# Handing tap products to the Pool engine in a fused convolution and two-layer feed-forward kernel

## The reference

```python
w = np.exp(weight_gen - max); w = w / (sum(w) + 1e-9)          # over the 7 taps
x_unf = x_pad[:, idx, :]...                                    # 7 tokens, this one and 6 before
x = np.einsum('bshk,bskhg->bshg', w, x_unf).reshape(B * S, D)  # 24 channels of each head
h = x @ w_in;  x = np.maximum(0.01 * h, h) @ w_out
h = x @ w_in2; r = np.maximum(h, 0.0); out = (r * r) @ w_out2
```

## Time and profile before

| | |
|---|---|
| median of three runs | 1122.15 us (1121.98, 1122.15, 1123.47) |
| the profiled execution | 1122.14 us, its span 1120.2 us |
| PE busy | 1114.8 us, 100% of the span |
| DVE, ACT, POOL busy | 873.2, 656.3 and 7.9 us |
| first matmul of the first `up` | at 11.30 us |

### The profile page before, as it was taken

How to read it: one execution, slowest core, us unless ns; L and a number is a source line. 1 busy time by engine, 2 the same in 40 slices (tenths; PEclk the granted TensorE clock), 3 DMA queues, 4 the chain that set the end, 5 groups by cost and what they waited for, 6 DMA issues and landing times.

```text
span 1120.2 us, 22873 instructions
## 1 busy us (share of the span) xinstructions
PE 1114.8 (100%) x9924; PEld 1108.4 (99%) x9924; DVE 873.2 (78%) x1051; ACT 656.3 (59%) x786; POOL 7.9 (1%) x14
## 2 busy tenths in 40 slices
PE   9999999999999999999999999999999999999998
PEld 8999999999999999999999999999999999999998
DVE  8898886978869787796877869778697786975575
ACT  6666656466565655655656565664656656566564
POOL 2000000000000000000000000000000000000000
PEclk9999999999999999999999999999999999999999
DMA  5311010100102001020010200102001020000001
GB/s 163 107 56 54 12 57 2 43 28 14 56 1 58 12 15 55 3 59 10 15 55 6 58 8 16 54 6 59 7 15 54 11 56 5 16 15 15 1 1 29
DMA packets 81059, 36.54 MB, mean 33 GB/s; under 512 B 58436, under 2 KB 78530, under 8 KB 80960
## 3 DMA queue, kind: packets, MB, share of 16 engines
q1 hardware_dynamic: 80960, 35.10, 11.9%
HBM read 23.25 MB, written 6.29 MB: 26 GB/s over the span
## 4 chain that ended last, share of the span: by engine, by line
PE 99%; DVE 0%; DMA 0%; ACT 0%; issue 0%; ACTq 0%; DVEq 0%
PE h_pair L1133 46%; PE y_main_psum L1178 31%; PE y_rest_psum L1182 21%; PE h_pair L1075 0%; PE h_pair L1142 0%; DMA tap_logits<-in_weight_gen_dram 0%; PE y_main_psum L1075 0%; DVE tap_product L725 0%; PE y_rest_psum L1206 0%; PE h_pair L1227 0%; DVE x_windows L949 0%; ACT x_windows L588 0%; ACT x_parts L491 0%; DVE tap_sum L705 0%; ACT tap_exp L485 0%
## 5 line engine op out<-in xcount | busy, mean ns | idle before, releaser
L1133 PE MATMUL h_pair<-x_parts,w_in_parts 64*128 64x512 f32 x4590 | 565.1, 386 | 0.0
L1133 PEld LDWEIGHTS h_pair<-x_parts,w_in_parts 64*128 64x128 f32 x4590 | 518.7, 184 | 1.7 <-issue 0.2
L1178 PE MATMUL y_main_psum<-g_hi,w_out_parts 64*128 64x512 f32 x2040 | 437.5, 386 | 0.0
L905 DVE TENSOR_TENSOR g_lo<-g,g_hi 128x1024 fp32r<-128x1024 f32 x255 | 311.1, 1220 | 126.1 <-ACT g_hi L574 96.0
L562 ACT ACTIVATE g_hi<-h_pair 128x1024 fp32r<-128x1024 f32 x126 | 129.6, 1029 | 191.8 <-PE h_pair L1133 191.7
L574 ACT ACTIVATE g_hi<-g 128x1024 fp32r<-128x1024 f32 x127 | 134.8, 1061 | 170.5 <-DVE g L896 170.5
L1178 PEld LDWEIGHTS y_main_psum<-g_hi,w_out_parts 64*128 64x128 f32 x2040 | 231.3, 184 | 0.8 <-issue 0.2
L1182 PE MATMUL y_rest_psum<-g_hi,w_out_parts 64*128 64x512 f32 x1020 | 218.7, 386 | 0.0
L1178 PE MATMUL y_main_psum<-g_lo,w_out_parts 64*128 64x512 f32 x1020 | 218.7, 386 | 0.0
L1182 PE MATMUL y_rest_psum<-g_lo,w_out_parts 64*128 64x512 f32 x1020 | 218.6, 386 | 0.0
L896 DVE SCALAR_TENSOR_TENSOR g<-h_pair,u 128x1024 f32<-128x1024 f32 x127 | 155.2, 1222 | 37.8 <-ACT u L568 36.0
(11 more groups left out here) (121 smaller groups left out, 428.6 us busy)
## 6 DMA issues: line engine op xcount, KB each, us to landing
x_windows<-in_x_dram SPq DMA_DIRECT2D x12, 960.0 KB
out_dram<-raw_w_in SPq DMA_DIRECT2D x360, 16.0 KB, 1.5
raw_w_in<-tap_product SPq DMA_DIRECT2D x336, 16.0 KB, 1.8
raw_w_out<-in_moe_w_out_dram SPq DMA_DIRECT2D x16, 192.0 KB, 3.9
tap_logits<-in_weight_gen_dram SPq DMA_DIRECT2D x16, 112.0 KB, 3.0
raw_w_in<-in_moe_w_in_dram SPq DMA_DIRECT2D x8, 192.0 KB, 3.4
raw_w_in<-in_moe_w_in_dram SPq DMA_DIRECT2D x8, 128.0 KB, 3.1
x_windows<-in_x_dram SPq DMA_DIRECT2D x2, 384.0 KB, 4.9
```

Source lines behind the costliest of these rows:

```text
L905: dve.tensor_tensor(GL[n % 4][:, :, :], gate[n % 2][:, :, :], GH[n % 4][:, :, :].bitcast(fp32), ALU.subtract).then_inc(glo_ready, 1)
L1133: last = pe.matmul(h[:, i, :], w[r, slot, a, c], v[r, slot, b, :], start=first, stop=end)
L1178: return pe.matmul(ym[rows][:, :], w[r, c], g[r, i, :], start=start, stop=stop)
```

## The change

Six things change. (1) POOL computes the weights of its own three taps of chunk 0, after DVE's reciprocal; DVE computes six of the seven weights for itself, and no longer the three for POOL. (2) For chunk 1 POOL makes the products of taps 6, 5 and 4 and adds them up in `SECOND[1]` (three products, two adds); DVE makes the four others and adds them in `SECOND[0]`, and at the end adds POOL's sum to it. The order of these operations in the steps of segment 0 is new. (3) `turn_second` turns one sum in place of two. (4) The main part of chunk 0's turned input is rounded half by ACT and half by DVE (`first_x_hi`). (5) The idle pair after the third turned product goes; the one at the end of `turn_first` stays. (6) The first two softmax operations of chunk 1 move on DVE from ahead of `in_lo(0)` to behind `in_lo(1)`.

```diff
+    POOL_SECOND = 3
+    SECOND_OPS = [("times", K - 1 - POOL_SECOND, 0)]
+    for t in range(K - 2 - POOL_SECOND, -1, -1):
+        SECOND_OPS += [("times", t, 2), ("plus", 0, 2)]
+    SECOND_OPS += [("plus", 0, 1)]
...
+            pool.wait_ge(ident_step, 4)
+            pool.wait_ge(conv_op, SOFT - 1)
+            which = slice(min(POOL_TAPS), K, 2)
+            pool.tensor_tensor(tap_w[:, :, which], tap_exp[:, :, which],
+                               tap_rec[:, :].unsqueeze(2).broadcast_to((P, TH, len(POOL_TAPS))), ALU.mult).then_inc(pool_weights, 1)
...
+            pool.wait_ge(x_hi_by_dve, 1)
             pool.tensor_copy(X[0][HP:P, 2, 0, :], X[0][0:HP, 0, 0, :]).then_inc(x_hi_spread, 1)
 
             pool.wait_ge(x_hi_spread, 2)
+            pool.wait_ge(first_loaded[1], 16)
+            pool.wait_ge(first_rest_turned, 1)
+            pool.wait_ge(conv_op, before(1) + SOFT)
+            for i in range(POOL_SECOND):
+                t = K - 1 - i
+                if i:
+                    pool.wait_ge(pool_second, 2 * i - 1)
+                pool.tensor_tensor((prod[1][:, :] if i else SECOND[1]).rearrange("p (a g) -> p a g", g=G),
+                                   xwin[1][:, t * D:(t + TPC) * D].rearrange("p (a g) -> p a g", g=G),
+                                   tap_w[:, :, t].unsqueeze(2).broadcast_to((P, TH, G)), ALU.mult).then_inc(pool_second, 1)
+                if i:
+                    pool.wait_ge(pool_second, 2 * i)
+                    pool.tensor_tensor(SECOND[1], SECOND[1], prod[1][:, :], ALU.add).then_inc(pool_second, 1)
...
-                main = X[s % 2][:, 0, 0, :].rearrange("p (a c) -> p a c", a=2)
-                act.activation(main, hb[pair][:, :, 0:QC], ACT.Copy).then_inc(x_hi_done, 1)
+                n = 1 if s == 0 else 2
+                main = X[s % 2][:, 0, 0, 0:n * QC].rearrange("p (a c) -> p a c", c=QC)
+                act.activation(main, hb[pair][:, 0:n, 0:QC], ACT.Copy).then_inc(x_hi_done, 1)
...
-                    weights(tap_w, slice(min(POOL_TAPS), K, 2)).then_inc(pool_weights, 1)
-                    return weights(first_tap_w, slice(0, K))
+                    return weights(first_tap_w, slice(0, K - 1))
...
+                    if b == 1:
+                        dve.wait_ge(pool_second, 2 * POOL_SECOND - 1)
...
+            def first_x_hi():
+                dve.wait_ge(x_turned, 1)
+                dve.tensor_copy(X[0][:, 0, 0, QC:NC], hb[PAIR[("first turn",)]][:, 1, 0:QC]).then_inc(x_hi_by_dve, 1)
...
                 if j == 0:
                     for i in range(2, SOFT):
                         softmax(1, i).then_inc(conv_op, 1)
-                    second_sums(range(2))
+                    second_sums(range(1))
                 if j == 1:
-                    second_sums(range(2, 4))
+                    second_sums(range(1, 2))
                     in_lo(2)
                 if j == 2:
                     out_lo(1)
+                    second_sums(range(2, 4))
+                if j == 3:
                     second_sums(range(4, 6))
-                if j == 3:
-                    second_sums(range(6, 8))
                     in_lo(3)
                 if j == 4:
                     out_lo(2)
-                    second_sums(range(8, len(SECOND_OPS)))
+                    second_sums(range(6, len(SECOND_OPS)))
...
             first_products()
-            for i in range(2):
-                softmax(1, i).then_inc(conv_op, 1)
             in_lo(0)
+            first_x_hi()
             x_lo_main(0, PAIR[("first turn",)])
...
             in_lo(1)
+            for i in range(2):
+                softmax(1, i).then_inc(conv_op, 1)
...
-                    if n in (2, K - 1):
-                        idle(1)
+                idle(1)
...
-                for b in range(2):
-                    last = turn_product(SECOND[b], main, rest, False, b == 0, b == 1)
-                last.then_inc(x_turned, 1)
+                turn_product(SECOND[0], main, rest, False, True, True).then_inc(x_turned, 1)
```

More of the change, by code:

```diff
@@ L251, in conv_two_ffn_kernel @@
         idle_ready = sem("idle_operand_ready")
+        pool_second = sem("pool_second_chunk_op")
+        x_hi_by_dve = sem("first_x_hi_done_by_dve")
         x_turned = sem("x_transposed")
@@ L460, in _ @@
             pool.wait_ge(x_hi_done, 1)
+            pool.wait_ge(x_hi_by_dve, 1)
             pool.tensor_copy(X[0][HP:P, 2, 0, :], X[0][0:HP, 0, 0, :]).then_inc(x_hi_spread, 1)
             pool.wait_ge(x_hi_spread, 2)
+            pool.wait_ge(first_loaded[1], 16)
[11 more added lines that the diff above has]
+                    pool.tensor_tensor(SECOND[1], SECOND[1], prod[1][:, :], ALU.add).then_inc(pool_second, 1)
+            pool.wait_ge(pool_second, 2 * POOL_SECOND - 1)
             pool.wait_ge(conv_op, before(NCH - FIRST_PLACE))
@@ L484, in exp_of @@
                 act.wait_ge(conv_op, before(k) + EXP + 1)
+                if k == 1:
+                    act.wait_ge(pool_weights, 1)
                 act.activation(tap_exp[:, :, 0:K], tap_shift[:, :, :], ACT.Exp).then_inc(exp_done, 1)
@@ L706, in softmax @@
                 if i == 3:
+                    if k == 1:
+                        dve.wait_ge(pool_weights, 1)
                     return dve.reciprocal(tap_rec[:, :], tap_sum[:, :])
@@ L801, in moved_lo @@
                 last.then_inc(moved_taken, 1)
+            def first_x_hi():
+                dve.wait_ge(x_turned, 1)
+                dve.tensor_copy(X[0][:, 0, 0, QC:NC], hb[PAIR[("first turn",)]][:, 1, 0:QC]).then_inc(x_hi_by_dve, 1)
             def x_lo_main(s, pair):
+                if s == 0:
+                    dve.wait_ge(x_hi_by_dve, 1)
                 dve.wait_ge(x_hi_done, 1 if s == 0 else 2 * s + 2)
@@ L1145, in first_up @@
                 pe.wait_ge(x_hi_done, 1)
+                pe.wait_ge(x_hi_by_dve, 1)
                 product(0, 0, 0, start=True)
```

## The result

The changed kernel takes 1128.38 us (median of six runs, 1128.27 to 1129.64) against 1122.30 for the kernel before. The ratio is 1.0055, with a 95% interval of 1.0042 to 1.0068. It is slower by about 6.1 us, clear of the 0.2% that counts here as no change, where I had forecast no change and 0.93 us less. Even the upper end of my range, 1127.3, was too low.

A forecast was written before the change was run, and what follows sets the result against it. PE was taken to bound the kernel. Gains of 0.38 (head), 0.50 (second turn) and 0.05 (third `down`) sum to 0.93 us, from 1122.14 to 1121.2 us; own range 1120.5 to 1122.4, whole range 1120.5 to 1127.3.

The forecast's parts named there:

- What bounds the kernel: PE, busy for the whole span; DVE is not the bound but has no room from 18 to 38 us.
- POOL in segment 0: Chunk 1's three products and two adds on POOL: 8.3 us, ending at 26.4, with over six us of cover.
- first rival: POOL and DVE hold each other up in segment 0, so PE waits: 1125 to 1127 us; chance 0.43.
- three forms: Engines take turns (chance 0.23), DVE always first (0.16), or slowing in part that stays inside the bound (0.04).
- 0.15 us overlap at 5.55: A POOL product started while a DVE operation with two SBUF inputs ran; no wait seen, judged to tell little.
- the clock: Second rival: without the idle pair at 8.57 PE's clock falls during the transposes, +1.95 us, 1123.2 in all; chance 0.04.
- The second turn: Turn of chunk 1: 16 transposes in place of 32, 1.00 becomes 0.50 us on PE's path, gain 0.50.
- The 0.05 at the third `down`: PE's wait for `out_lo(1)` at 26.54 goes, as DVE has two operations fewer ahead of it: 0.05 us gained.
- The head: Start of the kernel up to `first_up`, which starts and ends 0.38 us earlier; between 0.45 earlier and 0.3 later.
- DVE's own head start: Chunk 0's weights on DVE: without POOL's and with 192 elements for 224, the next operation starts 0.23 us earlier.
- POOL's weights: POOL's 128x96 weight operation for chunk 0: 0.35 us estimated, first product starting at 5.75, 0.20 later than before.
- third rival: POOL's third product holds up `in_lo(0)` by 0.3 to 0.4 us, delaying DVE's rounding: 0.38 gone, 1121.6; chance 0.05.

The follow-up runs named there:

- e2: The kernel before plus only POOL's three taps of chunk 1, the new order of DVE's sums and the single turn; 1128.69 us, ratio 1.0055.
- e3: The changed kernel with POOL's five operations on chunk 1 replaced by ten memsets of the same tiles; 1121.55 us, ratio 0.9992.
- e6: The changed kernel with POOL's five operations on chunk 1 replaced by eight copies with one SBUF input each; 1123.76 us, ratio 1.0012.
- e1: The changed kernel without POOL's work on chunk 1, which DVE convolves alone and which is turned as two sums; 1122.32 us, ratio 0.9999.
- e4: The changed kernel with chunk 1 convolved by DVE alone into one sum, one add more, turned once; 1121.47 us, ratio 0.9992.
- e9: The changed kernel with DVE's gate_lo, in_lo and out_lo in segment 0 moved ahead of chunk 1's sums; 1124.53 us, ratio 1.0017.

## Why the prediction was wrong, point by point

**What bounds the kernel** was read rightly, and so was the place of danger: DVE full from 18 to 38 us, with PE waiting for what it makes.

**The step that failed** is "POOL in segment 0": a price of 1.55 us an operation, 8.3 us in all, hidden behind six us of cover, and nothing charged to DVE. In its place the operations took 2.15 to 2.67 us, 12.2 from first start to last end, and DVE lost 1.35 to 1.6 us at each of five meetings, 7 us in all, against 3.8 taken off it. e2 shows that it is this part, e3 and e6 that it is POOL's reading.

I had the mechanism as the first rival, with the right order, and it came out as worked out: `in_lo(2)` at 26.7 (measured 26.48), `out_lo(1)` at 32.1 (31.52), waits of 2.6 and 3.3 (2.2 and 2.8). That it came so near is in part luck: I left out the start-up of 0.13 to 0.15 us that runs beside the other engine, and took 1.55 for an add that ends 1.67 behind DVE. The mistake was the choice. I gave it 0.43 in three forms and the forecast 0.44, on "no run shown decides it". But the kernel itself held a hint that I named and did not weigh: chunk 0's weights for DVE lie in PSUM, and the only stretch in which both engines worked at once was built so. One of those products in the timeline before the change, beside POOL's of 1.55 at 5.55:

```profile
6.62 0.95 DVE L725 TENSOR_TENSOR g<-x_windows,h_pair 128x768 f32<-128x768 f32 x1
```

The absence of slowing there was evidence about DVE operations with one input in SBUF alone. The 0.15 us overlap at 5.55 was too short to speak, since 0.13 to 0.15 us of an operation are start-up that runs beside the other engine anyway.

**The range** failed by a second term that I had at another place: the clock. I priced it for the removed idle pair, at 1.95 us; there it did not fall (the stretches of e1, e4 and the changed kernel all read 1.00 up to 18 us, and, since that figure also stood beside the 625 ns matmuls of the start, `first_up` itself says more: it takes 2.45 us in the changed kernel, 2.52 before). It fell behind the waits of the first rival, for 1.62 us. The rival's time should have been 1127.1 + 1.6 = 1128.7, and the range with it. The measured 1128.4 lies below that because the two waits together came out 0.9 us shorter than worked out, while the head gained 0.3 less and the late `down` cost its 0.21.

**The second turn** gained what was said, 0.50 (0.45 to 0.53 in the chain). **The 0.05 at the third `down`** can't be seen in the changed kernel. In e3_pool_writes_only, where nothing collides, that pair took 0.23 in place of 0.28, as said.

**The head**: said 0.38, measured 0.09 (`first_up` ends at 13.73, before at 13.82). In this execution the logits landed later, and DVE's reciprocal began at 4.82 against 4.75 before, so an estimate of the head's own worth from these rows is 0.16. DVE's own head start came to 0.21 (5.21 to 5.61, before 5.13 to 5.74), near the 0.23 that I took. My two terms for it, 0.27 and 0.03, add up to 0.30, which was wrong: before the change the first weight operation ran to 5.40 and the second had started at 5.32. POOL's weights took 0.49, not 0.35, and its first product began at 5.96, not 5.75. Timeline of POOL and DVE in the changed kernel:

```profile
5.33 0.49 POOL L451 TENSOR_TENSOR tap_weights<-tap_exp,tap_reciprocal 128x96 f32<-128x96 f32 x1 [3.37 <-DVE tap_reciprocal L737]
5.96 1.54 POOL L461 TENSOR_TENSOR conv_out<-x_windows,tap_weights 128x768 f32<-128x768 f32 x1
...
8.96 1.03 POOL L461 TENSOR_TENSOR g<-x_windows,tap_weights 128x480 f32<-128x480 f32 x1
```

```profile
5.21 0.37 DVE L741 TENSOR_TENSOR h_pair<-tap_exp,tap_reciprocal 128x192 f32<-128x192 f32 x1
...
9.64 1.16 DVE L704 TENSOR_TENSOR w_in_parts<-raw_w_in,w_in_parts 128x768 fp32r<-128x768 f32 x1
10.73 0.41 DVE L838 CAST x_parts<-h_pair 128x256 fp32r<-128x256 f32 x1
```

DVE's weights (two SBUF inputs) run to 5.58, inside POOL's, which end 0.24 behind them, at 5.82. If the two take turns here too, POOL's operation has 0.24 + 0.13 = 0.37 us of its own, an estimate close to the 0.35 that I took. The mechanism of the third rival came true as well: POOL's last product ends at 9.99, `in_lo(0)` behind it takes 1.16 in place of 0.95 and ends at 10.80, and DVE's half of the rounding starts at 10.73, where `x_turned` had let ACT begin at 10.59. In the traces of e1 and e4 a third thing covers whatever is left: a load that landed later, so that ACT's `out_hi(0)` ran from 10.21 or 10.49 and the rounding behind it began at 10.97 or 11.24. The chain of both goes through that DMA.

## What to carry to other kernels

Before work goes to POOL beside a full DVE, ask of each DVE operation how many of its inputs lie in SBUF: two inputs and a reading POOL means that the two take turns. Each of POOL's five operations held DVE up by 1.35 to 1.6 us here, and together they took four operations of 0.95 off it. A trace in which both run undisturbed proves nothing about this if there one input of DVE's was in PSUM. And when a rival makes PE wait for some us, its range should go up to the price with the slower clock behind the wait.

## What the runs showed of the hardware that I had not expected

- The alternation is strict and for whole instructions, even where DVE had its next operation ready: POOL was never starved, and a DVE operation of 0.42 us waited 1.6 us for its turn (2.02 in all).
- A POOL copy with one SBUF input shuts DVE out as well, for 0.62 us of 768 elements; ten memsets don't at all.
- An add of 768 elements ended on POOL 1.67 us behind DVE's end (23.99 to 25.66), a product with a broadcast weight 1.41 (21.76 to 23.17).
- The granted clock fell after two waits of 2.2 and 2.8 us with one `up` between them, to matmuls of 0.68 us, for 1.62 us of loss. It also fell with a single wait of 2.1 us (e2) and of 1.8 us (e9), and did not with one of 1.7 us (e6). It is visible as granted clock here, while the 625 ns matmuls of the start have a granted clock of 1.00 beside them. The earlier trace rows begins at 18 us, so here is the stretch of the kernel before:

```profile
2.00:4.00 2.00, 2.00 (x12) 1.57 (x10) 0.78 (x2) 0.28 (x2) 0.00 (x0) 1.00 0.94 236
```
